# Attention with a mixture of experts and an MLP: another order of the attention's steps, and other places for weight loads and stores

## The reference

```python
# 1. attention over the last 64 positions; 4 batches, 8 heads, 576 positions, 64 per head
scores = scale * q @ k.T            # masked to 0 <= row - column < 64
attn = exp(scores - max); attn /= attn.sum() + 1e-9
x = (attn @ v)                      # laid out as 2304 tokens x 512
# 2. experts: a token with x @ w_skip <= 0 keeps its x
e = argmax(x @ w_gate)              # one of 8 experts, gate = its softmax share
x += gate * (relu(x @ w1[e]) @ w2[e])       # 512 -> 1024 -> 512
# 3. MLP: h = x @ w_in (512 -> 2048); g = h * clip(h + 3, 0, 6) / 6; out = g @ w_out
```

## Time and profile before

| | |
|---|---|
| median of 3 runs | 697.95 us (695.5 to 698.37) |
| the profiled execution | 697.97 us |
| its span, first to last instruction | 696.3 us |
| mean granted TensorE clock | 0.993 |
| first scores of tile 0, of tile 17 | 9.6 us, 111.7 us |
| first product of the experts | 137.3 us |

### The profile page before, as it was taken

How to read it: one execution, slowest core, us unless ns; L and a number is a source line. 1 busy time by engine, 2 the same in 40 slices (tenths; PEclk the granted TensorE clock), 3 DMA queues, 4 the chain that set the end, 5 groups by cost and what they waited for, 6 DMA issues and landing times.

```text
span 696.3 us, 17352 instructions
## 1 busy us (share of the span) xinstructions
PE 663.1 (95%) x6782; PEld 576.7 (83%) x6782; DVE 250.3 (36%) x810; ACT 241.5 (35%) x569; POOL 71.4 (10%) x121
## 2 busy tenths in 40 slices
PE   5997998689999999899999999999999999999998
PEld 4776776668887888899899989998999899989996
DVE  1676776201211112465442224222422242233222
ACT  3786786011121112464432223222322232223221
POOL 4233453301111111000000000000000000000000
PEclk9999999999999999999999999999999999999999
DMA  7999989598486172464220002000200020001001
GB/s 150 226 210 255 220 221 339 150 359 308 151 316 218 37 270 85 138 165 122 91 92 0 1 1 90 0 0 0 90 0 0 0 90 0 0 0 47 0 1 45
DMA packets 97347, 78.13 MB, mean 112 GB/s; under 512 B 61889, under 2 KB 76997, under 8 KB 97296
## 3 DMA queue, kind: packets, MB, share of 16 engines
q1 hardware_dynamic: 85056, 47.39, 25.3%
q10 hardware_dynamic: 9792, 25.83, 10.5%
q0 software_dynamic: 2448, 4.22, 1.8%
HBM read 63.23 MB, written 17.52 MB: 116 GB/s over the span
## 4 chain that ended last, share of the span: by engine, by line
PE 80%; DMA 8%; DVE 5%; ACT 2%; issue 2%; SPq 2%; POOLq 0%; POOL 0%; DVEq 0%; ACTq 0%
PE bank L752 29%; PE bank L765 19%; PE av L765 10%; PE av L726 7%; PE bank L715 7%; DMA xin<-x_rows 4%; DVE sm L959 3%; PE bank L581 2%; DMA kraw<-in_k 2%; PE bank L630 1%; SPq L361 1%; DVE xall L972 1%; ACT pr L811 1%; PE av L686 1%; PE av L737 1%
## 5 line engine op out<-in xcount | busy, mean ns | idle before, releaser
L907 ACT ACTIVATE rel<-bank,half 128x384 f32<-128x384 f32 x96 | 55.7, 580 | 185.8 <-PE bank L752 185.8
L1093 DVE SCALAR_TENSOR_TENSOR act<-rel,bank 128x384 f32<-128x384 f32 x96 | 53.2, 554 | 169.8 <-ACT rel L907 169.7
L752 PE MATMUL bank<-xT_hi,wi_hi 128*128 128x384 f32 x384 | 83.3, 339 | 0.7 <-ACT xT_hi L900 0.7
L752 PE MATMUL bank<-xT_hi,wi_lo 128*128 128x384 f32 x384 | 82.9, 337 | 0.0
L752 PE MATMUL bank<-xT_lo,wi_hi 128*128 128x384 f32 x384 | 82.0, 334 | 0.0
L1097 DVE TENSOR_TENSOR g_lo<-act,g_hi 128x384 fp32r<-128x384 f32 x96 | 53.6, 558 | 67.2 <-ACT g_hi L918 67.2
L765 PE MATMUL bank<-wo_hi,g_lo 128*128 128x512 f32 x192 | 76.2, 397 | 0.0
L765 PE MATMUL bank<-wo_hi,g_hi 128*128 128x512 f32 x192 | 76.1, 396 | 0.0
L765 PE MATMUL bank<-wo_lo,g_hi 128*128 128x512 f32 x192 | 75.8, 395 | 0.0
L752 PEld LDWEIGHTS bank<-xT_hi,wi_hi 128*128 128x128 f32 x384 | 69.0, 188 | 7.6 <-ACT xT_hi L900 0.9
L918 ACT CAST g_hi<-act 128x384 fp32r<-128x384 f32 x96 | 49.3, 513 | 64.9 <-DVE act L1093 64.9
(11 more groups left out here) (122 smaller groups left out, 796.4 us busy)
## 6 DMA issues: line engine op xcount, KB each, us to landing
w1s<-in_moe_w ACTq DMA_DIRECT2D x6, 2048.0 KB, 9.2
w2s<-in_moe_w ACTq DMA_DIRECT2D x6, 2048.0 KB, 15.3
qraw<-in_q SPq DMA_DIRECT2D x36, 128.0 KB
kraw<-in_k SPq DMA_DIRECT2D x36, 128.0 KB
vnow<-in_v SPq DMA_DIRECT2D x36, 128.0 KB, 4.1
x_new<-xall SPq DMA_DIRECT2D x18, 256.0 KB
out<-ot SPq DMA_DIRECT2D x18, 256.0 KB, 2.2
xn<-x_new SPq DMA_DIRECT2D x17, 256.0 KB, 3.6
```

Of the source, the lines that this page charges most:

```text
L752: last = pe.matmul(bank[f % 4][:, 0:GN], a[:, f, c, :], b[:, c, :], start=(n == 0), stop=(n == 3 * DC - 1))
L907: sc.activation(rel[f % 2][:, :], bank[f % 4][:, 0:GN], ACT.Relu, scale=1.0 / 6.0, bias=half[:, :]).then_inc(s_rel, 1)
L1093: dve.scalar_tensor_tensor(out=act[f % 2][:, :], in0=rel[f % 2][:, :], scalar=1.0, in1=bank[f % 4][:, 0:GN], op0=ALU.min, op1=ALU.mult).th ...
```

## The change

PE now transposes q and k for tiles 0 and 1 ahead of the loop, and in step T those of tile T+2; `qT` gets a third buffer. The probabilities of tile T are transposed in step T+1, just ahead of their product with v. transpose_xs and logits move from one and two steps behind the scores to two and three, transpose_lg from two to four, and the logits go to bank 5. `choose` moves to the steps with T % 3 = 0 and from the end to just before `normalise`; `ranks`, `place` and the exponent `lex` move to the steps with T % 3 = 1 from step 7 on, and `place` stands right after take_scores, ahead of DVE's take_logits(T-4), take_k(T+2) and normalise(T-1). PE's values(T-1) waits for that take_logits(T-4). The loop has two steps more. Stores are issued six tiles behind in place of three. Expert 0's first four pieces are issued in iterations 3, 7, 11 and 15, its last four in iteration 17; expert 1's weights go in two issues of 2 MB onto ACT's queue in its step 18; expert 2's are issued when expert 0 is done, ahead of expert 3's. The idle turns use 8 fp32r matmuls of 256 columns in place of 16 bf16 ones of 128.

```diff
-        qT = [put("W", f"qT{i}", [P, HP, P]) for i in range(2)]
+        qT = [put("W", f"qT{i}", [P, HP, P]) for i in range(3)]
...
+        warm = sb("warm", [P, 2 * P], fp32r)
...
+        STORE = 6
...
             if e < 2:
-                eng.wait_ge(s_w[e], 8 * 16)
+                eng.wait_ge(s_w[e], (8 if e == 0 else 2) * 16)
...
-            for T in range(1, NT + 3):
+            for T in range(1, NT + STORE):
                 if T < NT:
                     load_v(T)
                 if T + 2 < NT:
                     load_qk(T + 2)
-                if T <= 2 * DC:
-                    weights_piece(sp, 0, T - 1)
+                if T >= STORE:
+                    store_x(T - STORE)
+                if T % DC == DC - 1 and T < NT:
+                    weights_piece(sp, 0, T // DC)
                 if T == NT - 1:
-                    for n in range(2 * DC):
-                        weights_piece(sp, 1, n)
-                if T >= 3:
-                    store_x(T - 3)
+                    for n in range(DC, 2 * DC):
+                        weights_piece(sp, 0, n)
...
-                if T >= 6:
-                    scatter(T - 6)
-            for T in range(NT - 6, NT):
+                if T >= 8:
+                    scatter(T - 8)
+            for T in range(NT - 8, NT):
                 scatter(T)
...
             def ranks(G):
...
-                pe.wait_ge(s_x, min(G * GT + 2 * GT - 1, NT))
+                pe.wait_ge(s_x, min(G * GT + 2 * GT, NT))
...
             def values(T):
...
                 if T >= 1:
                     pe.wait_ge(s_x, T)
-                if T >= 2:
-                    pe.wait_ge(s_lgc, T - 1)
-                if T >= 2 * GT - 1:
-                    pe.wait_ge(s_rkc, (T - 2 * GT + 1) // GT + 1)
+                if T >= 3:
+                    pe.wait_ge(s_lgc, T - 2)
+                if T >= 2 * GT:
+                    pe.wait_ge(s_rkc, T // GT - 1)
...
             def transpose_pr(T, a):
...
                 if T >= 2 and a == 0:
-                    pe.wait_ge(s_lgs, T - 1)
+                    pe.wait_ge(s_xtc, T - 1)
+                if T >= 3 and a == 1:
+                    pe.wait_ge(s_lgs, T - 2)
...
             def logits(T):
...
                 pe.wait_ge(s_xtc, T + 1)
+                pe.wait_ge(s_prc, 2 * min(T + 3, NT))
+                if T == NT - 1:
+                    pe.wait_ge(s_lgs, T)
                 for c in range(DC):
-                    last = pe.matmul(bank[4][c * LW:(c + 1) * LW, 0:P], wg[:, c, :], xsT[T % 2][:, c, :],
+                    last = pe.matmul(bank[5][c * LW:(c + 1) * LW, 0:P], wg[:, c, :], xsT[T % 2][:, c, :],
...
             def transpose_xs(T):
                 pe.wait_ge(s_x, T + 1)
-                if T + 1 < NT:
+                if T + 2 <= NT:
                     pe.wait_ge(s_prc, 2 * T + 3)
                 else:
-                    pe.wait_ge(s_lgs, T)
+                    pe.wait_ge(s_xtc, T)
...
             def transpose_lg(T):
                 pe.wait_ge(s_lgs, T + 1)
-                pe.wait_ge(s_x, min(T + 2, NT))
-                if T == NT - 1:
+                pe.wait_ge(s_x, min(T + 3, NT))
+                if T >= NT - 2:
                     pe.wait_ge(s_lgc, T)
...
             transpose_qk(0)
-            for T in range(NT + 3):
+            transpose_qk(1)
+            for T in range(NT + 5):
                 if T < NT:
                     scores(T)
+                if exists(T - 4, NT):
+                    transpose_lg(T - 4)
+                if T % GT == 1 and T >= 2 * GT + 1:
+                    ranks(T // GT - 2)
+                if exists(T - 1, NT):
+                    transpose_pr(T - 1, 0)
+                    transpose_pr(T - 1, 1)
+                if T + 2 < NT:
+                    transpose_qk(T + 2)
+                if exists(T - 2, NT):
+                    transpose_xs(T - 2)
+                if exists(T - 3, NT):
+                    logits(T - 3)
                 if exists(T - 1, NT):
                     values(T - 1)
-                if exists(T - 2, NT):
-                    logits(T - 2)
-                if T + 1 < NT:
-                    transpose_qk(T + 1)
-                if T < NT:
-                    transpose_pr(T, 0)
-                if T % GT == 2 and T >= 2 * GT - 1:
-                    ranks((T + 1) // GT - 2)
-                if exists(T - 2, NT):
-                    transpose_lg(T - 2)
-                if T < NT:
-                    transpose_pr(T, 1)
-                if exists(T - 1, NT):
-                    transpose_xs(T - 1)
...
             def idle_turns(n):
                 with pe.Fori(0, n):
-                    for m in range(16):
-                        pe.matmul(bank[5][:, 0:P], before[:, :], ones[:, :], start=True, stop=True)
-
+                    for m in range(8):
+                        pe.matmul(bank[0][:, 0:2 * P], warm[:, 0:P], warm[:, :], start=True, stop=True)
...
             take_q(0)
-            for T in range(NT + 3):
+            take_q(1)
+            for n in range(2):
+                sc.copy(warm[:, n * P:(n + 1) * P], ident[:, :]).then_inc(s_warm, 1)
+            for T in range(NT + 5):
+                if exists(T - 1, NT):
+                    take_pr(T - 1, 0)
+                    take_pr(T - 1, 1)
+                if T == NT:
+                    load_w1(sc, 1, s_w[1])
+                    load_w2(sc, 1, s_w[1])
                 if T < NT:
                     exponents(T, 0)
-                if exists(T - 2, NT):
-                    take_logits(T - 2)
+                if exists(T - 3, NT):
+                    take_logits(T - 3)
                 if T < NT:
                     exponents(T, 1)
-                    take_pr(T, 0)
-                if T + 1 < NT:
-                    take_q(T + 1)
-                if T < NT:
-                    take_pr(T, 1)
-                if T % GT == 2 and T >= 2 * GT - 1:
-                    sc.wait_ge(s_dl, (T + 1) // GT - 1)
+                if T % GT == 1 and T >= 2 * GT + 1:
+                    sc.wait_ge(s_dl, T // GT - 1)
                     sc.activation(lex[:, :, :], ldl[:, :, :], ACT.Exp).then_inc(s_lex, 1)
-                if exists(T - 1, NT):
-                    take_xs(T - 1)
+                if exists(T - 2, NT):
+                    take_xs(T - 2)
+                if T + 2 < NT:
+                    take_q(T + 2)
...
             sc.wait_ge(s_scat, 16 * NT)
-            load_w1(sc, 2, s_wp1[2])
-            load_w2(sc, 2, s_wp2[2])
             for e, first, end in expert_tiles(sc, bounds):
...
                     fixed(sc)
+                    if e == 0:
+                        load_w1(sc, 2, s_wp1[2])
+                        load_w2(sc, 2, s_wp2[2])
                     load_w1(sc, e + 3, s_wp1[e % 3])
                     load_w2(sc, e + 3, s_wp2[e % 3])
...
             def take_k(T):
                 dve.wait_ge(s_qkt, T + 1)
+                if T >= 3:
+                    dve.wait_ge(s_klow, T - 1)
...
             take_k(0)
-            for T in range(NT + 3):
+            take_k(1)
+            for T in range(NT + 5):
                 if T < NT:
                     take_scores(T)
+                if T % GT == 1 and T >= 2 * GT + 1:
+                    place(T // GT - 2)
+                if exists(T - 4, NT):
+                    take_logits(T - 4)
+                if T + 2 < NT:
+                    take_k(T + 2)
+                if T % GT == 0 and T >= 2 * GT:
+                    if T == 2 * GT:
+                        dve.wait_ge(s_const, 1)
+                    choose(T // GT - 2)
                 if exists(T - 1, NT):
                     normalise(T - 1)
-                if T + 1 < NT:
-                    take_k(T + 1)
-                if exists(T - 2, NT):
-                    take_logits(T - 2)
-                if T % GT == 1 and T >= GT + 1:
-                    if T == GT + 1:
-                        dve.wait_ge(s_const, 1)
-                    choose((T - 1) // GT - 1)
-                if T % GT == 2 and T >= 2 * GT - 1:
-                    place((T + 1) // GT - 2)
```

More of the change, by code:

```diff
@@ L211, in attention_moe_mlp_kernel @@
         s_tbl = sem("s_tbl")
+        s_warm = sem("s_warm")
         s_pad0 = sem("s_pad0")
@@ L581, in scores @@
                             last = pe.matmul(bank[2 + p][x * W:(x + 1) * W, j * KH:(j + 1) * KH],
-                                             qT[T % 2][rows, j, x * W:(x + 1) * W],
+                                             qT[T % 3][rows, j, x * W:(x + 1) * W],
                                              kT[T % 3][rows, j, 0:3:2, :] if x else kT[T % 3][rows, j, 0:2, :],
@@ L691, in idle_turns @@
                 with pe.Fori(0, n):
-                    for m in range(16):
-                        pe.matmul(bank[5][:, 0:P], before[:, :], ones[:, :], start=True, stop=True)
+                    for m in range(8):
+                        pe.matmul(bank[0][:, 0:2 * P], warm[:, 0:P], warm[:, :], start=True, stop=True)
```

(5 more changed lines are left out.)

## The result

The changed kernel takes 716.53 us (median of 4, 715.23 to 718.75) where the kernel before takes 698.16 (median of 4, 695.5 to 700.52): a ratio of 1.0268, interval 1.0222 to 1.0313. It is slower, as forecast, but by 18.4 us and not by 11; 716.5 lies outside the range of 694 to 715. The profiled execution had 716.1 us and a span of 714.5.

A forecast was written before the change was run, and what follows sets the result against it. Late attention was taken as bound by a 5.67 us loop through PE, DVE and ACT plus load waits, experts and MLP by PE. Terms 12.9 - 1.5 - 1.0 - 4.6 + 4.8 - 4.5 + 1.0 + 4.0 = +11.1 gave 709 us, range 694 to 715.

The forecast's parts named there:

- Place steps, +12.9: Attention steps 7, 10, 13, 16: PE's values waits 2.9 us behind place and lex; 3.2 us more each, bounds 9 to 14.
- Clock, +4.0: PE's clock falls to half behind the new waits in four place steps, 1.0 us each; bounds 0 and 6.8.
- Ordinary steps, -1.5: Nine attention steps without place, from tile 4 on, take 5.5 us where 5.67 before; bounds -3 and +3.
- Steps 0 to 3: First attention steps: expert 0's pieces are gone but all still wait for loads; -1.0 us, give or take 1.
- Load waits, -4.6: Attention tiles 5 to 17: the 5.2 us of waiting for loads go except 0.6; bounds -5.2 and 0.
- Tail, +4.8: After tile 17's scores: its values start 8.8 us later, last logits reduction at 15.8 where 11.0 before; 3 to 6.
- Experts, -4.5 + 1.0: Expert stage: first tile's load wait and slow clock go, -4.5; expert 2's weights, issued after expert 0, land late, +1.0.
- the gate's wait is covered: Rival, place steps: ACT reaches lex early enough that values(T-1) waits for nothing; about 692 us, chance 0.18.
- half covered: Rival, place steps: PE's wait behind the gate is halved; 699 us, chance 0.07.
- Late loads: Rival, attention: landing exceeds 4.7 us, so every other ordinary step waits about 1 us; 714 us, chance 0.10.

The follow-up runs named there:

- the repeat: The changed kernel, unchanged, run and traced a second time on another set's chip: 718.8 us, ratio 1.029 to the kernel before.
- before_again: The kernel before, unchanged, run and traced again on the same chip as the changed kernel's second run: 697.21 us.
- e2_first: The changed kernel with expert 2's weights issued before the first expert tile, as in the kernel before: 720.8 us, ratio 1.0223.
- e3_on_pool: The changed kernel with expert 3's weights issued by GpSimd at the end of expert 0, expert 2's staying with ACT: 730.01 us, ratio 1.0361.
- before_third: The kernel before, unchanged, a single run beside the second run of the moved transfers alone: 706.81 us.

## Why the prediction was right or wrong

**Place steps, +12.9, right in mechanism, undersized.** Its chain is the measured one link by link, and the wait of 2.9 came as 3.11, 2.93, 2.93 and 3.22. It takes 9.4 per step where 8.9 was said. What is off in this term is "makes it late by 0.3": `choose` took 2.3 us there against 1.47 in the earlier trace rows, and the transpose of logits came 2.44 after scores, not 1.7. All that follows is late by the same 0.7: pos 8.0 for 7.3, the reduction 8.1 for 7.5, values 8.5 for 7.8.

**Clock, +4.0, partly.** The bounds of 0 and 6.8 hold. In the first trace three of the four waits left the clock at 1.00, and only that of tile 16 brought it to 0.50; in the repeat three of four fell. Single microseconds of the first (PE busy (x), PEclk, DMA share, GB/s), ahead and behind the waits that end at 56.44 and 116.28:

```profile
55.00:56.00 1.00, 0.00 (x0) 1.00 1.05 276
56.00:57.00 1.00, 0.56 (x19) 1.00 0.34 118
57.00:58.00 1.00, 1.00 (x37) 1.00 0.00 0
...
115.00:116.00 1.00, 0.00 (x0) 1.00 0.91 296
116.00:117.00 1.00, 0.72 (x14) 0.54 0.94 320
117.00:118.00 1.00, 1.00 (x24) 0.50 1.08 274
```

And of the repeat:

```profile
57.00:58.00 1.00, 1.00 (x24) 0.50 0.00 0
58.00:59.00 1.00, 1.00 (x23) 0.50 0.06 16
```

In the repeat it fell in the steps of tiles 7, 10 and 16, and not in that of 13. The price of one is 1.05 in the step of tile 7 (10.66 against 9.61) and 0.61 in that of tile 10 (10.04 against 9.43), so at most what the estimate of 1.0 had. The error was to take it four times for certain. With the place steps' 9.4 in sum, clock and all, the two terms came to 4 x 3.75 = +15.0 against 16.9 in the first trace, and to +16.8 in the repeat. The Trainium skill, "TensorE: Matmul & The Clock Gate", section on HAM oscillation, describes a loop whose clock drops in every pass, at its wait for data; here it fell behind one such wait in four and behind three in four, in two executions of one program.

**Ordinary steps, -1.5.** 5.26, not 5.47: nine of them make 9 x (5.26 - 5.67) = -3.7, just past the bound of -3. Steps 0 to 3 gave -0.65 for -1.0.

**Load waits, -4.6, right.** Past tile 4 one wait of 1.05 for k is left of 5.2, so -4.1. It is right for the changed order with its idle 12 us of PE, in which loads have time. The experiments show that the two terms aren't independent: take the gate's wait away, and up to 6.8 us of waiting for k come. Nor is it the placing of the transfers alone that brings it, since that brought nothing in the old order. These terms sum to -0.65 + 15.0 - 3.7 - 4.1 = +6.6, the measured difference at tile 17.

**Tail, +4.8, right in the first trace.** Values of tile 17 start 9.2 after its scores (8.8 forecast), the last reduction comes at 16.5 (15.8), the whole is +5.7, within 3 to 6. In the repeat it is +7.1, outside, with the values of tile 17 at half clock: the prediction had no clock term for the tail.

**Experts, -4.5 + 1.0, wrong, and the step that failed.** The first half held: expert 2's weights no longer run beside the first tile, and the second tile's rows aren't late. The sentence that failed is "its second half lands 15.3 after issue, issued 0.4 to 0.9 later: +1.0". It asked when the bytes land, and they landed in 15.0 (median). It did not ask how long ACT is held while it issues four loads, nor what stands behind them. The kernel before issues only two such loads in a row, and the earlier trace rows show 0.38 for the first of each pair; I took four to be twice two. Measured: 5.2 of waiting for hT and 2.8 by the slow product behind it, where +1.0 (0 to 3) stood. To that come 1.6 by the first product at half clock (5.50 where it took 3.95 before) and a pause of 0.8 at 186: 10.4 - 4.5 = 5.9, against +6.0 in the table. Without the hold and the slow clock behind it the measured difference would be 18.3 - 8.0 = 10.3, and the time, near 708, inside the range. In the repeat the same two items are 6.0 + 2.8 = 8.8, and the gain on the other side is larger, since the second tile's rows had been late by 3.85 in before_again: 8.8 - 3.85 - 1.7 = 3.3 against a measured +2.7. There too 18.4 - 8.8 = 9.6 would lie inside. But the range was missed by 1.5 us only, so a smaller excess elsewhere, such as the tail of the repeat, could tip it as well; and these are estimates, since no kernel took the hold away alone: e2_first paid with late rows, e3_on_pool with a late expert 2.

**Rivals.** That the gate's wait is covered, or half covered, is excluded by the 12.2 us. Late loads was right in kind for a kernel without the gate's wait, and not in this one. That an issue could hold its engine was no rival, and it should have been one: here an engine in the path got four large issues in a row, where it had got two.

**Open.** Why the third and the fourth issue are long was not tried: loads of half the size, or other instructions between, would tell. Nor is it known what decides whether the clock falls in waits so alike, or why the same kernel takes some 5 us more in the experts on one chip (142.7 against 137.9), where each tile's first product takes 4.1 to 4.3 us in place of 3.9 at full clock and the profile shows nothing that it waits for.

## What to carry to other kernels

When a load is moved, price not only when its bytes land but how long its issuing engine is held, and name the instruction behind it; where the list of before shows two large issues in a row and the change makes four, the cost of the last two is unknown and belongs in the range. In an order written by hand, look at the smallest instruction at the head of a long wait: one exponent of 0.22 us, standing behind eight others, held up four waits of 3 us, and moving it alone gave most of that back. A wait that is removed speeds up the engine that others feed, so price the next wait (here k, behind the load of v) along with it. And before a difference is cut into stages, look at a second pair of traces: here the sum repeated to 0.1 us and its parts did not.

## What was unexpected of the hardware

- Loads of 2 MB issued by ACT one after another: the first two held it 0.39 and 0.85 us, the third and fourth 3.73 and 2.99. Over all eight traces with late weights the third held it 3.73 to 5.06 us, the fourth 2.68 to 3.08, and PE waited 5.1 to 6.4. Two alone took 0.38 and mostly 0.53, the second 1.59 at the most.
- Two queues with 4 MB each share the engines: PE began the expert that was wanted first 26.7 us after its last issue, where such a load lands in 15.0 otherwise.
- Waits of PE of 2.9 to 3.3 us, equal to the eye, brought the granted clock to 0.50 behind some and not behind others, and in another execution of the same program behind other ones.
- The same kernel took 697 us on one chip and 707 on another (before_again and before_third; medians there 698.73 and 705.38), with its end of the experts at 273.95 and 283.44.
